# Splitting the second weight matrix of the next expert one tile later

## The reference

```python
x = attn_out.transpose(0, 2, 1, 3).reshape(3072, 512)
e_idx = np.argmax(x @ w_gate, axis=1)
for e in range(8):
    mask = e_idx == e
    h = np.maximum(x[mask] @ w1[e], 0.0)      # w1[e]: 512 x 1024
    ye = h @ w2[e]                            # w2[e]: 1024 x 512
    out[mask] = gate_w[mask, None] * eom[mask, e, None] * ye
```

## Time and profile before

| | |
|---|---|
| median of 3 runs | 1160.51 us (1159.92 to 1163.32) |
| the profiled execution | 1156.39 us, span 1154.6 us |
| PE busy | 1117.5 us, 97% of the span |
| ACT busy, DVE busy | 383.0 us (33%), 437.6 us (38%) |
| mean granted clock of PE | 0.992 |

### The profile page before, as it was taken

One profiled execution on the slowest core, in us unless ns is written; L12 is line 12 of the kernel. 1 busy time (PEld: TensorE's weight loads), 2 busy tenths in 40 slices (PEclk: granted clock), 3 DMA queues, 4 the chain that ended last, 5 costly groups with the idle time before them and its releaser, 6 DMA issues.

```text
span 1154.6 us, 19327 instructions
## 1 busy us (share of the span) xinstructions
PE 1117.5 (97%) x6051; PEld 936.4 (81%) x6052; DVE 437.6 (38%) x826; ACT 383.0 (33%) x631; POOL 166.0 (14%) x216
## 2 busy tenths in 40 slices
PE   7999999999999999998999999999999999999995
PEld 6999988787878887876888788888888888888884
DVE  4777755432414416331434323222332332333221
ACT  2455433443434436432241313213131321313111
POOL 2444423333311101110000100100010010001001
PEclk9999999999999999998999999999999999999998
DMA  9989814534334633422200200100010010000000
GB/s 206 254 231 241 215 56 155 178 114 127 109 109 139 207 109 110 159 81 90 84 26 1 74 1 1 73 0 0 0 73 0 0 73 0 0 0 37 1 1 36
DMA packets 111838, 97.24 MB, mean 84 GB/s; under 512 B 80640, under 2 KB 86192, under 8 KB 111792
## 3 DMA queue, kind: packets, MB, share of 16 engines
q1 hardware_dynamic: 97744, 66.07, 20.7%
q0 software_dynamic: 7648, 22.60, 5.5%
q10 hardware_dynamic: 6400, 7.96, 2.1%
HBM read 76.40 MB, written 20.21 MB: 84 GB/s over the span
## 4 chain that ended last, share of the span: by engine, by line
PE 52%; ACT 0%; DVE 0%; issue 0%; POOLq 0%; POOL 0%; ACTq 0%
PE bank L660 17%; PE bank L662 17%; PE bank L661 17%; PE bank L631 0%; DVE hl L1279 0%; ACT hh L936 0%; POOLq L97 0%; POOL out_rows L1446 0%; ACT more_rows L943 0%; POOLq L1450 0%; ACTq L935 0%; POOLq L1445 0%
## 5 line engine op out<-in xcount | busy, mean ns | idle before, releaser
L1270 DVE TENSOR_TENSOR gated<-bank,sig 128x512 f32<-128x512 f32 x72 | 49.8, 692 | 323.0 <-ACT sig L929 323.0
L660 PE MATMUL bank<-xh,w1h 128*128 128x512 f32 x384 | 149.4, 389 | 0.0
L661 PE MATMUL bank<-xl,w1h 128*128 128x512 f32 x384 | 149.4, 389 | 0.0
L662 PE MATMUL bank<-xh,w1l 128*128 128x512 f32 x384 | 149.4, 389 | 0.0
L929 ACT ACTIVATE sig<-bank 128x512 f32<-128x512 f32 x72 | 43.1, 598 | 289.7 <-PE bank L662 289.7
L660 PE MATMUL bank<-w2h,hh 128*128 128x512 f32 x288 | 113.2, 393 | 4.7 <-DVE hl L1279 4.7
L662 PE MATMUL bank<-w2h,hl 128*128 128x512 f32 x288 | 112.2, 390 | 0.0
L661 PE MATMUL bank<-w2l,hh 128*128 128x512 f32 x288 | 112.1, 389 | 0.0
L1088 DVE TENSOR_TENSOR hidl<-bank,hidh 128x512 fp32r<-128x512 f32 x58 | 39.8, 687 | 151.1 <-ACT hidh L804 151.1
L1446 POOL DMA_INDIRECT out_rows<-x_out,cur_idx x12 | 11.8, 982 | 591.1 <-ACT x_out L943 589.3
L936 ACT ACTIVATE hh<-prod 128x512 fp32r<-128x512 f32 x72 | 45.5, 632 | 154.2 <-PE bank L662 133.6
(11 more groups left out here) (214 smaller groups left out, 1966.8 us busy)
## 6 DMA issues: line engine op xcount, KB each, us to landing
stage<-in_moe_w SPq DMA_DIRECT2D x64, 512.0 KB, 5.3
expert_rows<-tile_o ACTq DMA_DIRECT2D x29, 256.0 KB
q_raw<-in_q SPq DMA_DIRECT2D x24, 256.0 KB, 5.5
k_raw<-in_k SPq DMA_DIRECT2D x24, 256.0 KB, 6.2
v_raw<-in_v SPq DMA_DIRECT2D x24, 256.0 KB, 3.5
yr<-expert_rows SPq DMA_DIRECT2D x5, 1024.0 KB, 5.7
stage<-in_moe_w_out SPq DMA_DIRECT2D x6, 512.0 KB, 3.3
stage<-in_moe_w_gate SPq DMA_DIRECT2D x5, 512.0 KB, 7.1
```

Of the source, the lines that this page charges most:

```text
L660: pe.matmul(out_ap, lh, rh, start=first, stop=False)
L661: pe.matmul(out_ap, lh, rl, start=False, stop=False)
L662: return pe.matmul(out_ap, ll, rh, start=False, stop=last)
L1270: v3.tensor_tensor(gated[:], bank[GV[f % 2][0]][:, :], sig[:], ALU.mult).then_inc(s["gated_done"], 1)
```

## The change

Three tables are worked out by DVE beside the old ones. `held` is 1 in the second tile of a run whose first tile has `go` = 1; `whole` is 1 where `go` is 1 and there is no second tile; the old `go` stays. In a tile with `go` only the four pieces of w1 are split (and all of w2 too where `whole` is 1). In the tile with `held` three pieces of w2 are split between `tile_result` and relu 0 and the fourth after the store. SP's loads and PE's stream have the same instructions as before. To make room for the tables, `meta` and `meta_idx` move to memory that `more_rows` uses later, and POOL waits for the read back before it loads the MLP's first rows.

```diff
+HELD_EARLY = PER + 3
...
             def expert_tile(a):
                 is_go = act.value_load(go[0:1, ds(a, 1)], min_val=0, max_val=1)
+                is_held = act.value_load(held[0:1, ds(a, 1)], min_val=0, max_val=1)
+                is_whole = act.value_load(whole[0:1, ds(a, 1)], min_val=0, max_val=1)
                 run = act.value_load(run_of[0:1, ds(a, 1)], min_val=0, max_val=EXPERTS - 1)
                 to = act.value_load(next_at[0:1, ds(a, 1)], min_val=0, max_val=HALF)
...
                 with act.If(is_go):
                     split_run_hi(turn, to, range(EARLY))
+                with act.If(is_held):
+                    split_run_hi(turn, to, range(PER, HELD_EARLY))
                 relu(a, 0)
                 relu(a, 1)
                 turned_hi_parts(a)
                 store_tile(a - 1)
                 with act.If(is_go):
-                    split_run_hi(turn, to, range(EARLY, RUN))
+                    split_run_hi(turn, to, range(EARLY, PER))
+                    with act.If(is_whole):
+                        split_run_hi(turn, to, range(PER, RUN))
+                with act.If(is_held):
+                    split_run_hi(turn, to, range(HELD_EARLY, RUN))
...
+            also(v3.tensor_scalar(real_f[:], numbers[0:1, :], end_e[0:1, EXPERTS - 1:EXPERTS], None, ALU.is_lt))
...
-            settle(v3.tensor_tensor(go[:], more_new[:], mlp_f[:], ALU.add), 2)
+            also(v3.tensor_tensor(stays_f[:], real_f[:], new_f[:], ALU.is_gt))
+            also(v3.memset(held_f[:], 0.0))
+            settle(v3.tensor_tensor(go_f[:], more_new[:], mlp_f[:], ALU.add), 4)
+            also(v3.tensor_copy(go[:], go_f[:]))
+            settle(v3.tensor_tensor(held_f[:, 1:], go_f[:, 0:TILES], stays_f[:, 1:], ALU.mult), 2)
+            also(v3.tensor_copy(held[:], held_f[:]))
+            also(v3.memset(whole[:, TILES:], 0))
+            settle(v3.tensor_tensor(whole[:, 0:TILES], go_f[:, 0:TILES], held_f[:, 1:], ALU.subtract), 3)
             dve.sem_inc(s["control_ready"], 1)
...
             pool.wait_ge(s["early_done"], 2)
+            pool.wait_ge(s["meta_in"], 16)
             pool.dma_start(x_rows[:].bitcast(U32), y_dram[0:2 * P, :].rearrange("(t p) d -> p t d", p=P))\
```

More of the change, by code:

```diff
@@ L130, in build @@
         row_idx = sb(ctx, "row_idx", [P, TILES + 1], U32)
-        meta = sb(ctx, "meta", [P, UNITS, 2])
-        meta_idx = sb(ctx, "meta_idx", [P, UNITS], U32)
         meta_back = sb(ctx, "meta_back", [P, UNITS, 2])
@@ L147, in build @@
         go_mlp = sb(ctx, "go_mlp", [1, TILES + 1], I32)
+        held = sb(ctx, "held", [1, TILES + 1], I32)
+        whole = sb(ctx, "whole", [1, TILES + 1], I32)
         flags = sb(ctx, "flags", [1, 2], I32)
@@ L184, in build @@
             pick = sb(over, "pick", [P, EXPERTS])
+            meta = sb(over, "meta", [P, UNITS, 2])
+            meta_idx = sb(over, "meta_idx", [P, UNITS], U32)
             over.enter_context(nc.sbuf_tensor("up_to_xg", [P, over_at + XG_AT - nc.sbuf_base], mybir.dt.uint8))
@@ L223, in build @@
                     for n in ("run_f", "exp_f", "new_f", "last_f", "more_f", "last_new", "more_new", "mlp_f"))
+                real_f, go_f, stays_f, held_f = (sb(route, n, [1, TILES + 1])
+                                                 for n in ("real_f", "go_f", "stays_f", "held_f"))
                 par_i = sb(route, "par_i", [1, 1], I32)
@@ L1149, in _ @@
             also(v3.tensor_scalar(real[:], numbers[0:1, :], end_e[0:1, EXPERTS - 1:EXPERTS], None, ALU.is_lt))
-            settle(v3.tensor_reduce(run_f[:], begun[0:1, :, :], X, ALU.add), 3)
+            also(v3.tensor_scalar(real_f[:], numbers[0:1, :], end_e[0:1, EXPERTS - 1:EXPERTS], None, ALU.is_lt))
+            settle(v3.tensor_reduce(run_f[:], begun[0:1, :, :], X, ALU.add), 4)
             also(v3.tensor_tensor(ctl[:], upto_e[0:1, :].unsqueeze(1).to_broadcast(per_a),
@@ L1199, in expert_tile @@
                 is_go = dve.value_load(go[0:1, ds(a, 1)], min_val=0, max_val=1)
+                is_held = dve.value_load(held[0:1, ds(a, 1)], min_val=0, max_val=1)
+                is_whole = dve.value_load(whole[0:1, ds(a, 1)], min_val=0, max_val=1)
                 run = dve.value_load(run_of[0:1, ds(a, 1)], min_val=0, max_val=EXPERTS - 1)
@@ L1204, in expert_tile @@
                     split_run_lo(RUN * (run + 1), to, range(EARLY))
+                with dve.If(is_held):
+                    split_run_lo(RUN * (run + 1), to, range(PER, HELD_EARLY))
                 turned_lo_parts(a)
                 with dve.If(is_go):
-                    split_run_lo(RUN * (run + 1), to, range(EARLY, RUN))
+                    split_run_lo(RUN * (run + 1), to, range(EARLY, PER))
+                    with dve.If(is_whole):
+                        split_run_lo(RUN * (run + 1), to, range(PER, RUN))
+                with dve.If(is_held):
+                    split_run_lo(RUN * (run + 1), to, range(HELD_EARLY, RUN))
             for a in range(1, LEAD):
```

## The result

In the runs made beside the prediction the changed kernel took 1153.8 us (median of 4, 1153.43 to 1156.48) and the kernel before 1161.45 us (median of 4, 1159.92 to 1163.32): ratio 0.9938, 95% interval 0.9916 to 0.9961.

A forecast was written before the change was run, and what follows sets the result against it. PE, busy 97% of the span, bounds the kernel, so only its stalls and low clock count. Terms -4.87 + 0.6 + 1.3 + 2.0 + 0.1 give about -1.0 us: 1159.5 us from a median of 1160.51, range 1156.5 to 1162.5.

The forecast's parts named there:

- the first term: PE's stalls for relu before tiles 4, 8, 12 and 26 all go: 4.87 us gained.
- The two remaining run switches: Run switches not among PE's five waits for relu; claimed to cost PE nothing.
- The cause of the late relu: At tile 8, ACT waited 3.41 us for w2's last piece, then 2.22 us passed until `tile_o`, including three table loads.
- The chain on DVE: Eight more instructions ahead of `hidl` of tile 1: 0.6 us lost, once; bounds 0.4 and 0.8.
- The loads at tile 22: Two added table loads on ACT's late path lengthen PE's wait before tile 22: 1.3 us lost.
- The new stall of tile 23: Both loads and three w2 copies ahead of relu 0 make PE wait in tile 23: 1.9 to 2.0 us lost.
- Tile 24: Two added loads move `tile_o` to 473.4 and PE to 474.5, when it is due: 0.1 us counted.
- The clock: Rival: the clock falls at tile 23's new stall too, costing 1.5 us, net +0.5, 1161.0 us; chance 0.25.
- The rival of the loads and `held`: `held` stays 0, no split moves, two loads lengthen five stalls, plus the chain: +7.1 us, 1167.6 us; chance 0.03.

The follow-up runs named there:

- the third chip: Unedited kernels profiled again on another chip: before 1161.26 us (median of 17) and 1161.68 (of 12), changed 1154.14 us, ratio 0.9939.
- without the copies: Changed kernel, but in tile 23 alone all four pieces of w2 are split behind the store: 1152.78 us, ratio to before 0.9926.
- the late load: SP loads the fourth piece of w2 one split later, on both kernels: before with it 1172.12 us, changed with it 1154.79 us.
- the kernel with `held` at 0: Changed kernel with every addition, but `held` comes out 0, so all eight pieces split in the first tile: 1168.23 us, ratio 1.0107.

## Why the prediction was wrong, and what in it was right

**The step that failed** is the size of the first term, and with it the way the sum was carried over to the runs: "So all four stalls should go: 1.84 + 1.19 + 0.96 + 0.88 = 4.87 us gained", and then "on the median of the runs, 1160.51, it is 1159.5". The four stalls did go. But 4.87 us was what they cost in one execution of 1156.39 us, and the runs that the forecast was measured against took 1160 to 1163. None of those runs was profiled; that they had more of the same cost is read from the third chip. There before takes 1161.3 us, the stalls at run switches are 8.1 and 8.3 us in two traces, two more switches (tiles 16 and 19) are among them, and falls of the clock behind a stall come on top, 1.4 us each, none in one trace and two in the other, one of these behind tile 12 and one behind tile 22. The changed kernel takes 1153.8 to 1154.1 us in all three measurements of it, since ACT waits for no landing in its tiles. With the load issued 1.13 us later, before was 10.1 us slower, and the changed kernel was at 1154.79 us, 0.7 to 1.0 us above its time on other chips. Where before is fast, at 1155.7 us, the change gained 1.8 us, near the forecast 1.0. The gap of 4 us between the profiled execution and the median stood in the table ahead of the prediction, and I took it for an offset that is the same before and after. It was in large part the very term that the change removes.

**The two remaining run switches**, which by the prediction "cost PE nothing": true of that trace, by less than 0.1 us. There the last copy began 9.08 and 9.04 us behind the tile's transposes, and from 12.50 - 3.37 = 9.13 us on PE waits. On the third chip they cost 0.2 to 0.7.

**The cause of the late relu** (ACT waits for the landing, then issues table loads) was right; moving the one piece that waits is enough.

**The chain on DVE**, 0.6 us: measured 0.63.

**The loads at tile 22**, 1.3 us: 0.74. Three loads in 2.01 us were read as 0.67 each, but that stretch is not three equal prices: with the fourth load it is 2.52 us and with the fifth 2.73. In the loop, two loads with the branches beside them took 1.33. The Trainium skill ("DMA: Bandwidth & Descriptors", Latency and other measured facts) gives a `tensor_load` a floor of about 600 ns. The added loads at tile 22, 0.51 and 0.21 us, undercut it, so the measurement decides, and the prediction's "this case's 2.01 us for three agree with it" does not hold for a single load.

**The new stall of tile 23**, 1.9 to 2.0 us: with and without the copies 16.66 (with the late load) and 14.75 us on one chip, so 1.9.

**Tile 24**, 0.1 us: nothing (13.41 against 13.51).

**The clock.** I had asked whether it falls at tile 23; it did not (1.00 from 460 on). What I had not priced is the longer wait before tile 22. Behind its 2.23 to 2.26 us in the kernel before, the clock fell in three of five traces: the step to tile 23 was 13.39 and 13.41 us without a fall and 14.79 to 14.92 with one. Behind the 2.96 to 3.00 us of the changed kernel and its variants it fell in all six traces, and behind 2.74 and 2.75 us in one of two. Without the copies, 14.75 us, the fall was no dearer than before; in the first trace after it was, 17.75 - 1.9 = 15.8. So the fall seems to come more often, which six traces don't prove, and costs 1.4 to 2.4 us. It is small beside the first point.

**The rival of the loads and `held`**, +7.1 us: measured +12.5. The stalls and the chain that it names came to 6.2 us; the rest are the two switches that had just been free, 2.5 us, and the clock.

With the terms as measured, the traces are accounted for. On the third chip: -8.1 + 0.6 + 0.7 + 3.2 (tile 23, 16.61 against 13.39) = -3.6, and the profiled executions went from 1157.69 to 1153.98, 3.7 us. With the second trace of before, whose 1161.37 us is near the median: -8.3 - 1.4 (the fall behind tile 12) + 0.7 + 0.7 + 1.8 (tile 23, 16.61 against 14.79) = -6.5, and from tile 0 to tile 27 it went from 352.7 to 346.2 us; the medians differ by 7.1. On the chip where before takes 1155.7 us: -5.0 + 0.7 + 0.7 + 3.0 = -0.6, and the spans went from 1154.9 to 1154.0, the median by 1.8. So on the third chip most of the gain is the landing and the rest mainly falls of the clock behind the stalls; for the runs that were not profiled the falls are argued from their clocks. Not settled is why the transfer takes longer on some chips than on others, nor which kind of chip the first trace came from: its execution took 1156.39 us while its fellows took 1160 to 1163.

## What to carry to other kernels

When the profiled execution is faster than the median of the runs, ask which wait in it could be longer in the others, before carrying its sum over. A wait that ends with a transfer's landing is the first suspect, and what one trace shows of it is one draw. A change that takes such a wait off the path gains all of its spread: this one gained 1.8 us in one measurement and over 7 in two others. And find the one piece that waits: moving the last of eight pieces freed the run switches as moving four did, and made no new stall in tile 23.

## What the runs showed of the hardware

The same program took 1155.7 us on one chip and 1161.3 and 1162.0 us on two others, medians of 23, 17 and 11 runs, while the changed kernel, without a wait for a landing in its tiles, took 1153.85 us on the first and 1154.14 on the second of them. From the issue of one load of 512 KB to the copy that waited for it, in the same place of the program, it was 4.69 us on the first chip and 5.29 and 5.38 on the second.

A fall of the clock to 1.2 GHz followed waits of PE of 2.06 to 2.26 us in some executions and not in others: behind the 2.23 us before tile 22 the granted clock was 0.62 in the first trace, and in two traces of the same kernel on other chips the step behind that wait had no time lost. A wait of 2.35 us in the kernel with `held` at 0 had no fall behind it. A wait of 2.96 us was followed by over six microseconds at the lower level, and waits of 1.58 and 1.67 us by none. The Trainium skill ("TensorE: Matmul & The Clock Gate", Part 1: The HAM clock gate) says that the clock is set by activity in a window that runs free of the kernel; that the same wait has both outcomes agrees with it.

At the head of a tile written out for itself, ACT took 2.01 us with three table loads, 2.52 with four and 2.73 with five. In the hardware loop two loads and the branches beside them took 1.33 us. Where ACT was idle anyway, as at the heads of most tiles, the two loads cost nothing: the changed kernel's steps there are 12.5 us.
